# Two-layer rational MLP behind a DFT: the reciprocal of Q by one VectorE instruction, and a fourth numerator buffer

## The reference

```python
X = np.fft.fft(np.fft.fft(x, axis=1), axis=2).real      # x: (2, 3008, 256)
h = X.reshape(6016, 256) @ w_in1; r = np.maximum(h, 0.0)
x2 = (r * r) @ w_out1                                   # w_in: (256, 2048), w_out: (2048, 256)
h = x2 @ w_in2
h2 = h * h; h3 = h2 * h
P = a[0] + a[1] * h + a[2] * h2 + a[3] * h3
Q = 1.0 + np.abs(b[0]) * np.abs(h) + np.abs(b[1]) * h2
g = P / (Q + 1e-06)
return g @ w_out2
```

## Time and profile before

| | |
|---|---|
| median of 2 runs | 1068.24 us (1068.15 to 1068.34) |
| the profiled execution's own time | 1066.06 us |
| its span in the trace | 1064.3 us |
| mean granted TensorE clock | 0.99 |
| busy: PE, DVE, ACT, POOL | 1024.4, 882.4, 889.0, 567.7 us |

### The profile page before, as it was taken

The page is one execution under the profiler, slowest core; times in us unless marked ns, Lnnn a source line. Parts: engine busy times, 40 slices in busy tenths (PEclk is TensorE's granted clock), DMA queues, the critical chain, the costliest instruction groups (busy, mean ns, idle before and its releaser), DMA issues.

```text
span 1064.3 us, 13867 instructions
## 1 busy us (share of the span) xinstructions
PE 1024.4 (96%) x5288; PEld 869.6 (82%) x5288; DVE 882.4 (83%) x836; ACT 889.0 (84%) x928; POOL 567.7 (53%) x302
## 2 busy tenths in 40 slices
PE   9999899999999999999999999999999999999776
PEld 8798778888888888888888888888888888888665
DVE  2466798988888888988988988988988888888877
ACT  2358899999998998998998999989989988888574
POOL 0227666556566565565565565565655655555332
PEclk9999999999999999999999999999999999999888
DMA  9764000001001001001001001001001001000000
GB/s 251 274 213 179 1 1 21 1 1 40 1 1 40 1 1 40 1 1 40 2 1 40 1 1 40 1 1 40 1 1 40 1 1 36 1 21 1 0 20 15
DMA packets 22580, 36.50 MB, mean 34 GB/s; under 512 B 1601, under 2 KB 17394, under 8 KB 21874
## 3 DMA queue, kind: packets, MB, share of 16 engines
q1 hardware_dynamic: 22514, 35.63, 10.3%
HBM read 23.78 MB, written 11.81 MB: 33 GB/s over the span
## 4 chain that ended last, share of the span: by engine, by line
PE 79%; ACT 8%; DVE 6%; issue 5%; POOL 1%; DMA 0%; DVEq 0%; ACTq 0%; SPq 0%; POOLq 0%
PE ps L738 41%; PE ps L729 20%; PE ps L764 7%; PE ps L753 5%; PE ps L681 3%; DVE den_s L600 2%; ACT g_value L481 2%; PE ps L701 2%; ACT seed_s L496 1%; PE ps L690 1%; ACT g_value L460 1%; ACT seed_s L499 1%; ACT out_s L512 1%; DVE g_value L601 1%; ACT minus_s L454 1%
## 5 line engine op out<-in xcount | busy, mean ns | idle before, releaser
L738 PE MATMUL ps<-g_hi,w_out_lo 128*128 128x512 f32 (+1 forms) x764 | 302.1, 395 | 26.5 <-POOL g_lo L418 17.3
L416 POOL CAST g_hi<-g_value 128x1024 fp32r<-128x1024 f32 (+1 forms) x94 | 96.8, 1030 | 397.6 <-DVE g_value L618 397.6
L738 PE MATMUL ps<-g_hi,w_out_hi 128*128 128x512 f32 (+1 forms) x764 | 300.8, 394 | 0.0
L738 PE MATMUL ps<-g_lo,w_out_hi 128*128 128x512 f32 (+1 forms) x764 | 299.0, 391 | 0.0
L418 POOL TENSOR_TENSOR g_lo<-g_value,g_hi 128x1024 fp32r<-128x1024 f32 (+1 forms) x94 | 223.8, 2381 | 7.5
L408 POOL TENSOR_TENSOR g_lo<-g_value,g_hi 128x1024 fp32r<-128x1024 f32 (+1 forms) x86 | 203.8, 2370 | 2.6 <-ACT g_hi L469 2.6
L738 PEld LDWEIGHTS ps<-g_hi,w_out_lo 128*128 128x128 f32 x764 | 145.5, 190 | 58.6 <-POOL g_lo L418 19.3
L600 DVE SCALAR_TENSOR_TENSOR den_s<-den_s,b_abs,ps 128x1024 f32<-128x1024 f32 x88 | 112.7, 1281 | 73.3 <-ACT g_value L481 73.2
L738 PEld LDWEIGHTS ps<-g_hi,w_out_hi 128*128 128x128 f32 x764 | 145.6, 191 | 29.4
L738 PEld LDWEIGHTS ps<-g_lo,w_out_hi 128*128 128x128 f32 x764 | 146.4, 192 | 25.7
L609 DVE SCALAR_TENSOR_TENSOR den_s<-den_s,seed_s 128x1024 f32<-128x1024 f32 x88 | 113.3, 1288 | 25.7 <-ACT seed_s L499 25.7
(11 more groups left out here) (79 smaller groups left out, 1792.9 us busy)
## 6 DMA issues: line engine op xcount, KB each, us to landing
x_s<-x SPq DMA_DIRECT2D x16, 384.0 KB, 7.6
out_t<-out_s SPq DMA_DIRECT2D x11, 512.0 KB, 3.0
w_out_unsplit_lo<-w_out SPq DMA_DIRECT2D x2, 2048.0 KB, 18.6
tw_s<-twiddle SPq DMA_DIRECT2D x1, 3012.0 KB, 18.6
y_hi_dram<-y_stage_hi SPq DMA_DIRECT2D x10, 256.0 KB, 3.1
y_lo_dram<-y_stage_lo SPq DMA_DIRECT2D x10, 256.0 KB, 3.3
y_hi<-y_hi_dram SPq DMA_DIRECT2D x10, 256.0 KB, 2.8
y_lo<-y_lo_dram SPq DMA_DIRECT2D x10, 256.0 KB, 3.1
```

The costliest lines, as they stand in the source:

```text
L738: last = nc.tensor.matmul(acc[:, mb, 0:n], w[a][:, f, mb * P:(mb + 1) * P], g[c][:, i, 0:n], start=(f == 0 and j == 0), stop=(f == FB - 1 ...
```

## The change

The estimate's tile `seed_s` and its two biases go, and a bias tile `q_const` with 1 + 1e-6 comes. ACT's `whole_q` adds it to Q in place, by an Identity activation, where the logarithm and the exponential were. VectorE's `reciprocal` waits for that, and is one reciprocal instruction in place of the two passes. The numerators have four buffers, the fourth as large as the estimate's tile was, and L481 waits for the product of unit m-4.

```diff
-NUM_BUFS = 3
+NUM_BUFS = 4
...
-            def seed_from_q(m):
-                den, seed = den_of(m), seed_of(m)
+            def whole_q(m):
+                den = den_of(m)
                 act.wait_ge(q_done, m + 1)
-                if m >= LAST:
-                    act.wait_ge(g2_done, m - 1)
-                else:
-                    after(act, rec_done, m)
-                nc.scalar.activation(seed, den, ACT.Ln, bias=ln_bias[:, 0:1],
-                                     scale=2.0 ** -LN_SHIFT).then_inc(ln_done, 1)
-                act.wait_ge(ln_done, m + 1)
-                nc.scalar.activation(seed, seed, ACT.Exp, bias=exp_bias[:, 0:1], scale=-1.0).then_inc(seed_done, 1)
+                nc.scalar.activation(den, den, ACT.Identity, bias=q_const[:, 0:1]).then_inc(q_whole, 1)
...
             def reciprocal(m):
-                den, seed = den_of(m), seed_of(m)
-                dve.wait_ge(q_done, m + 1)
-                dve.wait_ge(seed_done, m + 1)
-                nc.vector.scalar_tensor_tensor(den, den, Q_CONST, seed, ALU.add, ALU.mult).then_inc(t_done, 1)
-                dve.wait_ge(t_done, m + 1)
-                nc.vector.scalar_tensor_tensor(den, den, 2.0, seed, ALU.subtract, ALU.mult,
-                                               reverse0=True).then_inc(rec_done, 1)
+                den = den_of(m)
+                dve.wait_ge(q_whole, m + 1)
+                nc.vector.reciprocal(den, den).then_inc(rec_done, 1)
```

## The result

The changed kernel takes 1325.56 us (1324.88 to 1326.23, 2 runs) against 1068.24 us: a ratio of 1.241, 95% interval 1.236 to 1.246. The forecast was slower, 1539 us in a range from 1235 to 1560. The direction and the mechanism were right; the length of the reciprocal was put at 8.68 us and is 6.54.

The account below looks back on a forecast made before the run. TensorE was taken as the bound before, VectorE after: 6.16 + 8.71 = 14.87 us a step, 85 steps 1264 us, ending at 1400.5 with small corrections; a drain of 124.0 and the tail led to 1539 us, range 1235 to 1560.

Parts of the forecast that it names:

- The bound: Steady state before the change: TensorE's matmuls are the period, 595.7 of 600 us busy; no other engine sets anything.
- VectorE's room of about 1.2 us a step: Steady steps: VectorE idles 1.19 of 9.91 us, so it can take about 1.2 us more before becoming the bound.
- the reciprocal's term: VectorE's reciprocal at 1024 elements: assumed eight passes at three bits each, 8.68 us; eight passes given 0.60.
- line for six passes: The case in which VectorE's reciprocal takes six passes: kernel time 1338 us; five to seven passes together given 0.20.
- The rest of VectorE's step: VectorE's work per step besides the reciprocal, after the two replaced passes go: 6.16 us.
- No new wait: VectorE before the reciprocal: the new wait for ACT's 1 + Q costs nothing, ready at 2.7 us and wanted at 3.8.
- The fourth buffer: Numerators: ACT may start a unit earlier, but ACT and TensorE are ahead anyway: 0, bound between -4 and 0 us.
- ACT's 1.24 us: ACT loses logarithm and exponential and gains an Identity, 1.24 us less a step: worth nothing, since ACT isn't the bound.
- Rival 3: TensorE's idle time lowers its clock: if all work ran slower, 1964 us; chance 0.06, shared with more than eight passes.
- Rival 1: VectorE's reciprocal runs in one to three passes: TensorE stays the bound, a drain gain gives 1057 us; chance 0.13.
- Rival 2: VectorE's reciprocal takes five to seven passes: VectorE is the bound but less so, 1238 to 1439 us; chance 0.20.

Follow-up runs that it names:

- e6: The kernel before with 15 more TensorE matmuls a unit as filler: 1219.37 us against 1065.79 in the same runs.
- e2: The changed kernel with the reciprocal on only the first half of each block's columns (128x512): 1067.48 us, 1.000 of the kernel before.
- e3: The changed kernel with the reciprocal on only three quarters of the columns (128x768): 1174.48 us, 1.101 of the kernel before.
- e7: The changed kernel without ACT's pass that adds 1 + 1e-6 to Q: 1324.99 us, 1.242 of the kernel before.
- e4: The changed kernel with ACT waiting for the product of unit m-3, so the fourth numerator buffer brings nothing: 1324.93 us, 1.242 of the kernel before.
- e9: The changed kernel with 15 more TensorE matmuls a unit as filler, only from unit 12 on: 1325.09 us, 1.242 of the kernel before.
- e1: The changed kernel with the reciprocal replaced by one plain VectorE pass of the same tile, inverse left out: 1051.96 us, 0.986 of the kernel before.
- e8: The changed kernel with one plain VectorE pass for the reciprocal and the wait for the product of unit m-3: 1060.18 us, 0.993 of the kernel before.
- e12: The changed kernel with its reciprocal taken on another tile, 128x384 bfloat16 ones, so Q isn't inverted: 1065.2 us in one run.

## Why the prediction was right in direction and too high

**The bound** before, right: e6. VectorE's room of about 1.2 us a step, right: e2 adds to VectorE 3.38 - 2.52 = 0.86 us a step and costs nothing; the changed kernel adds 6.57 - 2.52 = 4.05 and costs 2.71 a step, so 1.34 of it fell into the room. e3 gives the same 1.34: it adds (6.57 - 1.60) - 2.52 = 2.45 and costs (1097.1 - 129.2 - 871.2) / 87 = 1.11.

**The step that failed** is the reciprocal's term: "as an estimate three bits a pass, eight passes, 8 x 1.066 + 0.148 = 8.68 us". Measured are 6.542 us at 1024 elements and 5.046 at 784. It is 88 x (8.68 - 6.54) + 8 x (6.68 - 5.05) = 201 us of the sum. What was wrong in it is the count of passes, not the price of one: with six the same formula gives 6 x 1.066 + 0.148 = 6.544 us. (That the instruction makes six passes inside is not shown; it only lasts as long as six.) No row of before could give the count, and the guess of bits a pass was mine. The prediction's own line for six passes was 1338 us, 12 above what was measured, but it had given five to seven passes 0.20 and eight 0.60. So the direction was safe, since any count above 3.3 passes gives it, while the time lies in the range only because the range was wide enough to take in the less likely case.

The prediction read two places of the Trainium skill for this price, and the trace agrees with neither reading: not with eight cycles an element (VectorE: DVE Perf Modes, section "First, the fixed hardware budget"), nor with one (Vector Engine (DVE) Microarchitecture Reference, section "Anatomy of a single slice"). Against the 1.04 ns of a plain pass, taken as one cycle, the 6.25 ns measured are six.

**The rest of VectorE's step**, 6.16 us, was 6.04: 85 x 0.12 = 10 us. I had subtracted the idle times from the period, but while an engine waits it also loses the overlap of one instruction with the next; in the changed kernel L585 starts 1.20 us after L599 (the timeline above). With both terms mended the sum gives 1539 - 201 - 10 = 1328 us, against 1325.6. The same overlap makes VectorE's room 1.34 us and not 1.2. (The prediction's 9.93 us of TensorE work a step is a mean of 600 us over 60 steps, while its 9.91 us is one ordinary step; 87 steps last 871.2 us, 10.01 each. Nothing hangs on it.)

**No new wait**, right: 0.0 us before 96 reciprocals, and e7. **The fourth buffer** at nothing, right: e4. **ACT's 1.24 us** at nothing, right: ACT is busy for 560.6 of 900 us.

**Rival 3, the clock:** the lower clock came (0.947) and costs no time (e9). **Rival 1** was wrong as a case and too small as a sum: e1 gives 1052 us where it had 1057. e8 shows that 8 of its 16 us are the buffer's, for which the prediction allowed 4. **Rival 2** is what happened, at the length of six passes.

## What to carry to other kernels

Before an instruction that divides is put on an engine, compare its length with that engine's idle time per step plus the passes that it replaces. Where another engine is the bound only the excess counts, and all of it (here a reciprocal of 3.34 us was free, and from 4.94 to 6.54 us each microsecond cost one). Where that engine itself is the bound, as in the drain, all of it counts (e2 against e1). Four cheap passes on two engines can beat one instruction that lasts as long as six on one. A wait that costs nothing where its engine is late (e4) can cost 8 us where it is not (e8), so buffers are judged anew after each change of the bound.

## What the runs showed of the hardware

VectorE's reciprocal takes 6.25 ns an element and 143 ns (e2, e3 and the changed kernel: 512, 768 and 1024 elements), where a plain pass costs 1.04 ns an element; e12's 384 bfloat16 ones lie on the same line. TensorE's granted clock was 0.59 in a stretch of 4 us behind a gap of 2.40 us, most of it at 1.2 GHz, and 1.00 behind another gap of 2.41 us; with filler that leaves gaps of 0.7 us on average before the h2 products (36.1 us in 55 waits in e9) its mean over the steady steps is 1.00.
